# Attention's product with the values in two unbroken runs a pair of heads, with VectorE's copies of it in later slots

## The reference

```python
# attention: batch 4, 8 heads, 576 positions, head dimension 64
scores = matmul(q, k.T) / sqrt(64)
x = (log1p(|i - j|) / log1p(max(i, 1)))[..., None]
bias = maximum(x @ w1 + b1, 0) @ w2              # one value per head, i, j
attn = softmax(scores + bias)                    # rows sum to 1 (+1e-9 below)
out = matmul(attn, v)                            # [4, 8, 576, 64]
# first layer: x is out as 2304 tokens of 512 features
h = x @ w_in                                     # 2048 wide
x = (h * cos(h)) @ w_out
# second layer
xn = x / sqrt(mean(x*x) + 1e-6) * rms_g
out = (silu(xn @ w_gate) * (xn @ w_val)) @ w_out # 1536 wide
```

## Time and profile before

| | us |
|---|---|
| median of 3 runs (1193.71 to 1194.73) | 1194.29 |
| the profiled execution | 1191.96 |
| its span, first to last instruction | 1190.1 |
| PE busy in the span | 1163.0 |
| DVE, ACT, POOL busy | 662.5, 493.2, 477.6 |

### The profile page before, as it was taken

How to read it: one execution, slowest core, us unless ns; L and a number is a source line. 1 busy time by engine, 2 the same in 40 slices (tenths; PEclk the granted TensorE clock), 3 DMA queues, 4 the chain that set the end, 5 groups by cost and what they waited for, 6 DMA issues and landing times.

```text
span 1190.1 us, 21722 instructions
## 1 busy us (share of the span) xinstructions
PE 1163.0 (98%) x7464; PEld 1079.9 (91%) x7464; DVE 662.5 (56%) x1554; ACT 493.2 (41%) x1032; POOL 477.6 (40%) x506
## 2 busy tenths in 40 slices
PE   5889999999999999999999999999999999999998
PEld 2367777777899999999999999999999999999998
DVE  7978888888889857566665786642020020200201
ACT  7977778778733433333333333112121111111211
POOL 0067777777775423425242453841111111111111
PEclk9999999999999999999999999999999999999999
DMA  6844435253134000000000010430000000000000
GB/s 198 286 130 150 153 99 179 82 191 102 45 110 127 15 1 1 0 0 0 0 0 0 0 53 18 133 89 28 1 13 14 0 26 0 0 26 0 26 0 27
DMA packets 46681, 69.10 MB, mean 58 GB/s; under 512 B 3857, under 2 KB 27569, under 8 KB 46641
## 3 DMA queue, kind: packets, MB, share of 16 engines
q1 hardware_dynamic: 46640, 68.61, 18.5%
HBM read 53.26 MB, written 15.34 MB: 58 GB/s over the span
## 4 chain that ended last, share of the span: by engine, by line
PE 61%; issue 28%; POOL 6%; DVE 2%; DVEq 1%; DMA 1%; ACT 0%; POOLq 0%; SPq 0%; ACTq 0%
PE banks L531 7%; PE banks L857 7%; PE banks L859 7%; PE banks L858 7%; PE bank L857 6%; PE bank L859 6%; PE bank L858 6%; PE bank L573 6%; PE bank L557 5%; POOL product_low L1469 5%; PE bank L579 2%; DVE hidden L237 1%; DVEq L237 1%; PE bank L553 1%; PE bias_ps L271 1%
## 5 line engine op out<-in xcount | busy, mean ns | idle before, releaser
L857 PE MATMUL banks<-x_high,w_high_rest 128*128 128x384 f32 x672 | 225.4, 335 | 0.0
L859 PE MATMUL banks<-x_high,w_low_rest 128*128 128x384 f32 x672 | 224.6, 334 | 0.0
L858 PE MATMUL banks<-x_low,w_high_rest 128*128 128x384 f32 x672 | 224.6, 334 | 0.0
L1469 POOL TENSOR_TENSOR product_low<-X,product_high 128x384 fp32r<-128x384 f32 x72 | 72.9, 1013 | 345.6 <-ACT product_high L1412 345.6
L1450 DVE TENSOR_TENSOR X<-X,banks 128x384 f32<-128x384 f32 x72 | 39.7, 552 | 299.6 <-PE banks L859 299.6
L1252 POOL TENSOR_TENSOR product_low<-g,product_high 128x384 fp32r<-128x384 f32 x96 | 103.2, 1075 | 221.4 <-ACT product_high L1125 221.2
L857 PE MATMUL bank<-product_high,w_high_rest 128*128 128x384 f32 x480 | 160.6, 335 | 0.0
L859 PE MATMUL bank<-product_high,w_low_rest 128*128 128x384 f32 x480 | 160.4, 334 | 0.0
L858 PE MATMUL bank<-product_low,w_high_rest 128*128 128x384 f32 x480 | 160.4, 334 | 0.0
L678 DVE CUSTOM_DVE_ANT_0 probs<-banks,bias 128x576 f32<-128x576 f32 (+1 forms) x160 | 119.6, 748 | 16.3 <-PE banks L531 7.4
L626 ACT ACTIVATE probs<-probs,by_row 128x576 f32<-128x576 f32 (+1 forms) x160 | 123.4, 771 | 8.8 <-DVE by_row L678 7.4
(11 more groups left out here) (118 smaller groups left out, 2516.0 us busy)
## 6 DMA issues: line engine op xcount, KB each, us to landing
raw_qk<-in_qk SPq DMA_DIRECT2D x32, 576.0 KB, 3.8
bias_scratch<-bias_stage SPq DMA_DIRECT2D x36, 288.0 KB, 3.2
bias<-bias_scratch SPq DMA_DIRECT2D x32, 288.0 KB, 3.3
w_raw<-in_w_out SPq DMA_DIRECT2D x28, 256.0 KB, 2.6
values<-in_v SPq DMA_DIRECT2D x16, 320.0 KB, 4.1
w_raw<-in_w_in SPq DMA_DIRECT2D x16, 256.0 KB, 2.8
out_t<-X SPq DMA_DIRECT2D x5, 768.0 KB, 3.6
w_raw<-in_w_gate SPq DMA_DIRECT2D x12, 256.0 KB, 3.0
```

The source lines that it names most:

```text
L857: nc.tensor.matmul(out, high, x_high, start=start, stop=False)
L858: nc.tensor.matmul(out, high, x_low, start=False, stop=False)
L859: return nc.tensor.matmul(out, low, x_high, start=False, stop=stop)
L1469: pool.tensor_tensor(sl[f % 2][:, :], s, sh[f % 2][:, :].bitcast(F32), ALU.subtract).then_inc(s_split, 1)
```

## The change

The four parts become two: `mix` issues all eight products and the last one of a half in one go. `MIX_SLOTS = (4, 9)` puts the first half in slot 4 and the second in slot 9 of the same pair. `KEEP_SLOTS = (6, 1)` puts DVE's copies in slot 6, and in slot 1 of the pair after. The waits of the two parts are joined in one place. The piece that stood in the closing stretch of the phase (second half of pair 14) now stands in slot 9 of pair 15.

```diff
--- before.py
+++ after.py
@@ -33,7 +33,7 @@
 HS = S // 2
 QPAD = NQ * P
 EXP_LAG, T_LAG = 1, 4
-MIX_SLOTS = (3, 5, 8, 0)
+MIX_SLOTS, KEEP_SLOTS = (4, 9), (6, 1)
 EARLY_TILES = 3
 
 
@@ -558,26 +558,23 @@
                                            ident[0:rows, 0:rows])
             last.then_inc(turned_ready, 1)
 
-        def mix(n, parity, half, part, first, mixed=mixed):
+        def mix(n, parity, half, first, mixed=mixed):
 
             queries = slice(half * HS, (half + 1) * HS)
-            if part == 0:
+            if half == 0:
                 pe.wait_ge(att.values_in[parity], n * 8 + (16 - 8 * parity))
-                pe.wait_ge(copied, n * TILES + (NQ + 3) if half == 0 else (n + 1) * TILES)
-                if mixed is att.mixed_end:
-                    pe.wait_ge(end_copied, PAIRS)
-                elif not (first and half == 0):
-                    pe.wait_ge(mixed_copied, n * 2 + half)
-            for c in ((0, 1), (2, 3))[part]:
+            pe.wait_ge(copied, n * TILES + (NQ + 3) if half == 0 else (n + 1) * TILES)
+            if mixed is att.mixed_end:
+                pe.wait_ge(end_copied, PAIRS)
+            elif not (first and half == 0):
+                pe.wait_ge(mixed_copied, n * 2 + half)
+            for c in range(NQ - 1):
                 for h in range(2):
                     nc.tensor.matmul(mixed[h * D:(h + 1) * D, 0:HS], values[parity][:, c, h, :],
                                      probs_t[parity][:, h, c, queries], start=(c == 0), stop=False)
-            if part == 1:
-                pe.wait_ge(end_copied, n + 1)
-                if half == 1:
-                    pe.wait_ge(last_end_copied, n + 1)
-                nc.tensor.matmul(mixed[:, 0:HS], values[parity][:, NQ - 1, :, :].rearrange("p h d -> p (h d)"),
-                                 probs_t_end[parity][:, queries], start=False, stop=True).then_inc(mixed_ready, 1)
+            pe.wait_ge(end_copied if half == 0 else last_end_copied, n + 1)
+            nc.tensor.matmul(mixed[:, 0:HS], values[parity][:, NQ - 1, :, :].rearrange("p h d -> p (h d)"),
+                             probs_t_end[parity][:, queries], start=False, stop=True).then_inc(mixed_ready, 1)
 
         def slot(n, parity, s, step, compute=True):
 
@@ -588,11 +585,8 @@
                     turn(n - 1, TILES - T_LAG + s, False)
             elif compute:
                 turn(n, s - T_LAG, step == 0)
-            if s == MIX_SLOTS[3]:
-                if step > 1:
-                    mix(n - 2, parity, 1, 1, False)
-            elif step > 0 and s in MIX_SLOTS:
-                mix(n - 1, 1 - parity, *divmod(MIX_SLOTS.index(s), 2), step == 1)
+            if step > 0 and s in MIX_SLOTS:
+                mix(n - 1, 1 - parity, MIX_SLOTS.index(s), step == 1)
 
         def pair(n, parity, step):
             for s in range(TILES):
@@ -606,8 +600,6 @@
             pair(m * 2, 0, 2)
             pair(m * 2 + 1, 1, 2)
         for s in range(T_LAG):
-            if s == MIX_SLOTS[3]:
-                mix(LAST - 1, 0, 1, 1, False)
             turn(LAST, TILES - T_LAG + s, False)
             if s == 0:
                 pe.wait_ge(biased, PAIRS * TILES)
@@ -615,8 +607,7 @@
             elif s == 2:
                 chunks.first_h(pe, 1)
         for half in range(2):
-            for part in range(2):
-                mix(LAST, 1, half, part, False, att.mixed_end if half else mixed)
+            mix(LAST, 1, half, False, att.mixed_end if half else mixed)
 
     @block.scalar
     def _(act):
@@ -724,9 +715,9 @@
                     invert(m, r)
                 if step > 0 and s == T_LAG - 1:
                     keep_end(n - 1, 1 - parity)
-                if step > 1 and s == MIX_SLOTS[3]:
+                if step > 1 and s == KEEP_SLOTS[1]:
                     att.keep_mixed(dve, n - 2, 1)
-                elif step > 0 and s == MIX_SLOTS[1]:
+                elif step > 0 and s == KEEP_SLOTS[0]:
                     att.keep_mixed(dve, n - 1, 0)
                 if made is not None:
                     made(s)
```

## The result

The kernel after takes 1200.86 us (median of 4 runs, 1200.05 to 1201.09), the kernel before 1194.0 in the runs beside it: a ratio of 1.0060, with a 95% interval from 1.0048 to 1.0073. The forecast was 1204.9, in a range from 1196 to 1213.

What follows compares the result with a forecast made beforehand. PE was taken to bound the kernel. Merges -4.5, first chain +12.3 and second +2.8 gave +10.6 us on the profiled 1191.96, so 1202.6; the runs' median is 2.3 higher, giving 1204.9, range 1196 to 1213.

Steps and rivals of the forecast that it cites:

- What bounds the kernel: Whole kernel: PE sets the pace, busy for 1163.0 of 1190.1 us at its upper clock, 2.4 GHz.
- DVE's idle time lay where nobody waits: Attention: DVE's 0.73 us wait at each copy delays no PE work, so removing it is worth nothing by itself.
- The merge, 0.15 each: Products with the values: joining two four-product pieces saves 0.15 us, 30 times in pairs 0 to 14, 4.5 us in all.
- Leaving the short tile's transposes costs the same whatever follows: Slots 3 and 8: 64-row transposes take 0.40 to a product, 0.39 to a score; counted as no gain.
- The drain of the tiling mode: Entries into the runs: the skill's rule, read alone, would promise more than 0.15 a merge; the forecast counted nothing extra.
- The first chain: Score 5 to score 9, behind slot 4's run: DVE 4.95 against PE 4.13, 0.82 late, 15 times, 12.3 us.
- 0.46 and a gap of 0.15: DVE's copy at slot 6, between score 5 and score 9: 0.46 us plus 0.15 before the next read.
- The second chain: Score 0 to score 4, behind slot 9's run: DVE 4.72 against PE 4.52, 0.20 late, 14 times, 2.8 us.
- The copies, priced by their place in the chain: DVE's copies, two slots later, now fall where DVE is short; each stretch behind a run counts 0.46 + 0.15 us.
- The lock, taken as nothing: DVE's scaling meeting POOL's subtraction: either nothing or 0.48 us at each of 29 chains; the forecast took nothing.
- The rivals: Four alternatives: merges alone 0.11; holes eating the saving 0.08; lock or ScalarE on top 0.13, broken run within that.
- the merges alone: Rival for both stretches behind runs: DVE early enough, only the 4.5 us saving remains, 1189.8 us; chance 0.11.

## Why the prediction was right, and its size too large

- **What bounds the kernel, and that DVE's idle time lay where nobody waits**: right. Moving the copies alone changed nothing in a steady pair.
- **The merge, 0.15 each**: right in the rows (2.09 the run), and a pair with one merge and no hole took 16.15 to 16.26 against 16.32. In the time of a whole kernel it gave 0.8 and 1.0 us of 2.2, by the medians of the two kernels with one merge.
- **Leaving the short tile's transposes costs the same whatever follows**: held. In the kernel after, pair 14's slot 3, which ends in them with a score behind, takes 1.16; before, up to the product, 1.15. The drain of the tiling mode that the Trainium skill states (TensorEngine Tiling (Array Packing), section Key Properties) gave nothing beyond the merge. A change of mode does show in the rows, but in a place that the change kept: from full 128-row transposes to a product it is 0.53 (254.87 to 255.40 before), to another score 0.35 (253.80 to 254.15), and a pair has two such entries before (slots 5 and 0) and after (4 and 9).
- **The first chain, 4.95 against 4.13, 0.82 late**: right in mechanism and place, mis-sized. The term that failed is the copy's, "0.46 and a gap of 0.15": it took 0.36. The gap was no part of the copy's price. It was a wait of DVE for score 5: that score's last matmul starts at 249.39, and the read at 249.90 is the 0.51 behind it that the prediction itself uses. And the copy's 0.46 overlaps the next operation by some 0.08 where nothing is waited for, even if the copy itself was:

```profile
330.62 0.46 DVE L352 COPY X<-bank 128x288 f32<-128x288 f32 x1 [0.88 <-PE bank L579]
331.00 0.54 DVE L1173 SCALAR_TENSOR_TENSOR angle<-turns,banks 128x384 f32<-128x384 int32 x1
```

These rows are of the kernel before, 0.38 from start to start. PE's own side was 4.20, not 4.13. So 0.47, which over 15 chains is 5.2 us less than forecast. That is more than the whole error of 3.7 between 10.6 forecast and 6.9 measured: the holes that the prediction took as nothing, in pair 15 above all, gave some of it back. That the error came out so small is in part luck.
- **The second chain, 0.20 late**: 0.13 to 0.25 in pairs 2 to 14 but for one with 0.36 (slots 3 and 4 together), right in size and only in part for the reason given. In pairs 2, 3, 12, 13 and 14 score 4 is punctual, DVE's chain being 4.4 to 4.5 with a copy of 0.35, and the loss is the transposes' wait for tile 0's scaling, made late by the lock between DVE and POOL. In most of the others it is some of both.
- **The copies, priced by their place in the chain**: right. One slot later gave back 5 us, another slot of the chain nothing, and an extra copy cost 5.5 us more inside than outside.
- **The lock, taken as nothing**: wrong. It costs up to 0.17 in slot 4 of the steady pairs, and in pair 15 it holds 0.9 of the 1.9 us of holes. In two experiments it took the place of the hole that had been closed. SBUF — State Buffer in the Trainium skill (section Who interferes with whom) names copies, casts and `tensor_scalar` on VectorE among those that can take the lock; scaling and cast were both seen held, in the rows above.
- **The rivals**: the merges alone came nearest with one merge, where the piece in slot 8 lets DVE catch up. Two runs a pair were in no arrangement tried as fast as the kernel before. Whether a place exists for both is open; a third score buffer was not tried.

## What to carry to other kernels

When an engine that never waits feeds one that needs more time for each item, what matters is how far apart the feeder's other work stands, not only its total: spread pieces are the follower's time to catch up. Before merging them, sum both engines from the first item behind the merged piece to the next point where the feeder waits, with the follower starting idle. And an operation's place in that sum is worth nearly its full duration (0.30 to 0.36 of 0.36 here), whatever the engine's busy share says. Price an operation from start to start, and only from rows where its follower did not wait for something else: the gap of 0.15 behind the copy was such a wait.

## What was not expected of the hardware

A DVE scaling or cast that begins inside a subtraction of POOL (L377, L383) was held up each time, by up to 1.2 us (1.47 for a cast of 0.33), and ended 0.2 to 0.3 behind POOL's, except where it began so late that its own 0.5 ran past that end. A cast on POOL (L373) goes either way: at 248.44 it held up the scaling, at 149.86 the scaling ran in its own 0.50 and the cast took 1.21. In both the scaling's row begins 0.17 behind the cast's, so which of the two will wait cannot be read from the order of the rows' starts, and a steady pair of 16.20 or 16.54 us hangs on it.
